# Seven block products in place of eight for the last matrix products, with the value products one step later and the loads of weights moved

## The reference

```
x  = attention(q, k, v)            # 8 heads of 64, a band of 96 keys and 8 global ones, bias by distance
x  = sum over 2 of 4 experts e:    # gate * softmax(causal, (x wq[e]) (x wk[e])') (x wv[e]) wo[e]
u  = x + (x' U V)'                 # rank 32, mixes the 768 tokens
out = u + relu(u w_ch1) w_ch2      # 512 -> 2048 -> 512
```

## Time and profile before

| | us |
|---|---|
| median of 3 runs (lowest, highest) | 459.03 (458.44, 459.3) |
| the profiled execution: its own time | 458.41 |
| its span, first to last instruction | 456.6 |
| PE busy, share of the span | 442.3 (97%) |
| DVE, ACT, POOL busy | 190.8, 167.1, 173.1 |

### The profile page before, as it was taken

How to read it: one execution, slowest core, us unless ns; L and a number is a source line. 1 busy time by engine, 2 the same in 40 slices (tenths; PEclk the granted TensorE clock), 3 DMA queues, 4 the chain that set the end, 5 groups by cost and what they waited for, 6 DMA issues and landing times.

```text
span 456.6 us, 8488 instructions
## 1 busy us (share of the span) xinstructions
PE 442.3 (97%) x3194; PEld 368.0 (81%) x3194; DVE 190.8 (42%) x616; ACT 167.1 (37%) x452; POOL 173.1 (38%) x243
## 2 busy tenths in 40 slices
PE   4999999999999999998999999999999999999996
PEld 3677777887787887767998888888888888888885
DVE  5799989455632733544352222212223122222112
ACT  4888788232553654656430111110112111111102
POOL 2667766924961365775212122222112111222210
PEclk9999999999999999999999999999999999999999
DMA  8899950110020011110102011111111032311003
GB/s 257 257 244 298 299 161 1 51 45 2 1 94 0 2 47 47 47 48 1 47 10 61 24 46 46 41 31 46 47 46 47 0 93 92 93 46 47 25 1 138
DMA packets 29949, 33.47 MB, mean 73 GB/s; under 512 B 9204, under 2 KB 19444, under 8 KB 29908
## 3 DMA queue, kind: packets, MB, share of 16 engines
q1 hardware_dynamic: 29474, 32.40, 24.0%
q10 hardware_dynamic: 434, 0.52, 0.3%
HBM read 29.77 MB, written 3.15 MB: 72 GB/s over the span
## 4 chain that ended last, share of the span: by engine, by line
PE 89%; DVE 4%; issue 3%; ACT 2%; DMA 1%; SPq 0%; POOL 0%; DVEq 0%; ACTq 0%
PE ps_s L1220 27%; PE ps_o L1220 25%; PE ps_t L1220 12%; PE ps_s L1451 5%; PE ps_o L1484 4%; PE ps_t L1467 4%; PE ps_o L1272 3%; PE ps_s L1239 3%; PE ps_t L1252 3%; DVE probT L865 1%; PE ps_o L1396 1%; ACT prob L604 1%; DMA kT<-in_k 1%; DVE prob L847 1%; DVE smin L847 0%
## 5 line engine op out<-in xcount | busy, mean ns | idle before, releaser
L492 POOL TENSOR_TENSOR fl<-fraw,fh 128x512 fp32r<-128x512 f32 x32 | 41.4, 1292 | 177.9 <-DVE fh L1162 177.9
L604 ACT ACTIVATE prob<-prob,smin 128x256 f32<-128x256 f32 (+3 forms) x144 | 77.7, 540 | 36.4 <-DVE smin L847 36.0
L796 ACT ACTIVATE hidh<-ps_o 128x768 fp32r<-128x768 f32 x32 | 26.0, 813 | 175.9 <-PE ps_o L1220 175.9
L1203 DVE SCALAR_TENSOR_TENSOR hidl<-ps_o,hidh 128x768 fp32r<-128x768 f32 x32 | 30.7, 958 | 92.6 <-ACT hidh L796 92.6
L541 POOL TENSOR_SCALAR prob<-prob,sinv,one 128x256 f32<-128x256 f32 (+1 forms) x96 | 50.6, 542 | 22.4 <-DVE sinv L878 22.4
L567 POOL TENSOR_SCALAR prob<-prob,sinv,gate 128x128 f32<-128x128 f32 (+5 forms) x48 | 34.0, 717 | 51.6 <-DVE sinv L898 51.5
L1220 PE MATMUL ps_s<-hidh,fl 128*128 128x512 f32 x128 | 50.4, 394 | 0.0
L1220 PE MATMUL ps_s<-hidl,fh 128*128 128x512 f32 x128 | 50.2, 392 | 0.0
L1220 PE MATMUL ps_s<-hidh,fh 128*128 128x512 f32 x128 | 49.7, 388 | 0.0
L1162 DVE CAST fh<-fraw 128x512 fp32r<-128x512 f32 x32 | 14.4, 450 | 66.8 <-PE ps_t L1220 66.8
L1220 PE MATMUL ps_o<-xh,w_late 128*128 128x512 f32 (+1 forms) x160 | 41.6, 334 | 0.0
(11 more groups left out here) (182 smaller groups left out, 978.3 us busy)
## 6 DMA issues: line engine op xcount, KB each, us to landing
fraw<-in_w SPq DMA_DIRECT2D x32, 256.0 KB, 2.7
wraw<-in_w SPq DMA_DIRECT2D x8, 512.0 KB, 3.4
kT<-in_k SPq DMA_DIRECT2D x16, 224.0 KB, 4.1
vN<-in_v SPq DMA_DIRECT2D x8, 384.0 KB, 4.9
out<-prob SPq DMA_DIRECT2D x12, 256.0 KB, 2.8
qT<-in_q SPq DMA_DIRECT2D x7, 384.0 KB, 3.8
vB<-in_v SPq DMA_DIRECT2D x8, 192.0 KB, 4.8
kT<-in_k SPq DMA_DIRECT2D x7, 128.0 KB, 3.9
```

The costliest lines, as they stand in the source:

```text
L492: return pool.tensor_tensor(lo, raw, hi.bitcast(F32), ALU.subtract)
L604: act.activation(prob_s, prob_s, ACT.Exp, bias=smin[:, col:col + 1], scale=-1.0, accum_out=ssum[:, col:col + 1]).then_inc(done, 1)
L796: act.activation(hidh[:, f % 2, :], ps_o[:, 0:S], ACT.Relu).then_inc(hidh_done, 1)
L1203: dve.scalar_tensor_tensor(hidl[:, f % 2, :], ps_o[:, 0:S], 0.0, hidh[:, f % 2, :].bitcast(F32), ALU.max, ALU.subtract).then_inc(hidl_done, 1)
```

## The change

**The block products.** The 512 x 128k by 128k x tokens product behind `second` and `whole` is cut in 2 x 2 blocks of weights (a11 to a22, 256 x 256 elements seen as 128 rows x 256) and of inputs (b11 to b22: 128 rows x 256 tokens), and done by Winograd's form of Strassen's scheme: 7 block products instead of 8, with 4 sums of weights (s1 to s4) and 4 sums of inputs (t1 to t4) made beforehand, and 7 sums of results behind. The 1536 tokens go through in three parts of 512 (the middle one spans the two batches). Each part has 9 "pairs" g: first wo with op, then 8 pairs of hidden blocks. Seven PSUM banks hold the seven products through a part; `ps_o[0:512]` is left for one hidden block.

For each pair and engine, in the order of its program:

- SP loads 512 KB of w2 (or wo) into `fraw` once the low parts of the pair two before are done.
- DVE: `weights_combined(g+2)`, four additions or subtractions 128 x 256 from `fraw` to `fraw`; `hidden_combined(g+1)`, four of 128 x 256 from `hraw` (or `o32`) to `t_raw`; `hidden_lo(g+1)`, 128 x 768; `combined_lo(g+1)`, 128 x 1024. In the last pair of a part it makes the six sums of 128 x 512 out of PSUM in place of `hidden_lo`.
- ACT: relu of two hidden blocks, 128 x 512 each, out of PSUM; `hidden_hi`, 128 x 768; `weights_hi(g+2)`, 128 x 1792; `combined_hi(g+1)`, 128 x 1024.
- POOL: the low parts of the seven weight blocks, one subtraction of 128 x 1792; and `sum_22`, one addition of 128 x 512 for a part.
- PE: hidden block (g+1, 0); two products; hidden block (g+1, 1); five products. A product is six matmuls of 256 columns. Products with a t block wait for `combined_lo`. In the first and the last pair of a part the order is END_ORDER.

**Attention.** `values` comes one step later (d-4), x with it, and the loop is one step longer. wk is loaded behind the third pair's keys and values, together with wq and wv; constants behind the fifth pair; wk, wq for the second heads and wo behind the last. POOL splits wk and wq between divisions (SPLIT_AT) and no longer before the first; ACT and DVE no longer split wq. POOL no longer splits wo, which now goes through the pairs.

```diff
+TOKENS, BLOCK = 512, 256
+PARTS = B * S // TOKENS
+PAIRS = FT // 2 + 1
+PRODUCTS = {1: ("a11", "b11"), 2: ("a12", "b21"), 3: ("s4", "b22"), 4: ("a22", "t4"), 5: ("s1", "t1"), 6: ("s2", "t2"),
+            7: ("s3", "t3")}
+ORDER, END_ORDER = (1, 2, 3, 5, 7, 6, 4), (1, 2, 6, 7, 5, 3, 4)
+SPLIT_AT = {13: 0, 16: 1, 19: 2, 22: 3}
...
 # SP
+                if g >= 2:
+                    sp.wait_ge(al_done, g - 1)
...
 # POOL
+                    if d in SPLIT_AT:
+                        split_weight(SPLIT_AT[d])
...
+            def sum_22(c):
+                pool.wait_ge(sum_step, SUMS * c + 3)
+                pool.wait_ge(copy_done, 2 * c + 2)
...
+                pool.tensor_tensor(y22, u3, c5, ALU.add).then_inc(y22_done, 1)
+            for g in range(N_PAIR):
+                pool.wait_ge(ah_done, g + 1)
+                lo_of(fraw[:, g % 2, 1:8, :], a_hi[g % 3], a_lo[g % 3]).then_inc(al_done, 1)
+                if g > PAIRS and g % PAIRS == 1:
+                    sum_22(g // PAIRS - 1)
+            sum_22(PARTS - 1)
 # ACT
+            for g in range(N_PAIR):
+                if last_of_part(g):
+                    copy_of(g // PAIRS, 1, c1)
+                    if g + 1 < N_PAIR:
+                        combined_hi(g + 1)
+                    copy_of(g // PAIRS, 5, c5)
+                    if g + 2 < N_PAIR:
+                        weights_hi(g + 2)
+                else:
+                    hidden_out(g + 1, 0)
+                    hidden_out(g + 1, 1)
+                    hidden_hi(g + 1)
+                    if g + 2 < N_PAIR:
+                        weights_hi(g + 2)
+                    combined_hi(g + 1)
 # DVE
+            def weights_combined(g):
+                a21, a11, a22, a12, s1, s2, s3, s4 = (fraw[:, g % 2, n, :] for n in range(8))
+                dve.wait_ge(f_in[g % 2], 16 * (g // 2 + 1))
+                dve.tensor_tensor(s1, a21, a22, ALU.add).then_inc(s_step, 1)
+                dve.tensor_tensor(s3, a11, a21, ALU.subtract).then_inc(s_step, 1)
+                dve.wait_ge(s_step, 4 * g + 1)
+                dve.tensor_tensor(s2, s1, a11, ALU.subtract).then_inc(s_step, 1)
+                dve.wait_ge(s_step, 4 * g + 3)
+                dve.tensor_tensor(s4, a12, s2, ALU.subtract).then_inc(s_step, 1)
...
+            def combined_lo(g):
+                dve.wait_ge(bth_done, g + 1)
+                dve.tensor_tensor(bt_lo[g % 2], t_raw, bt_hi[g % 2].bitcast(F32), ALU.subtract).then_inc(btl_done, 1)
...
+            for g in range(N_PAIR):
+                if g + 2 < N_PAIR:
+                    weights_combined(g + 2)
+                if g + 1 < N_PAIR:
+                    hidden_combined(g + 1)
+                if not last_of_part(g):
+                    hidden_lo(g + 1)
+                    combined_lo(g + 1)
+                else:
+                    sum_11(g // PAIRS)
+                    if g + 1 < N_PAIR:
+                        combined_lo(g + 1)
+                    other_sums(g // PAIRS)
 # PE
-                    if d >= 3:
-                        values(d - 3)
+                    if d >= 4:
+                        values(d - 4)
...
+            for g in range(N_PAIR):
+                order = END_ORDER if g % PAIRS in (0, PAIRS - 1) else ORDER
+                ahead = not last_of_part(g)
+                if ahead:
+                    hidden(g + 1, 0)
+                pe.wait_ge(al_done, g + 1)
...
+                for k, n in enumerate(order):
+                    if k == 2 and ahead:
+                        hidden(g + 1, 1)
+                    last = product(g, n)
```

More of the change, by code:

```diff
@@ L770, in _ @@
                 first_mixed_hi(n)
+            weights_hi(0)
             w01_hi(4)
@@ L773, in _ @@
             w01_hi(5)
+            combined_hi(0)
             mixed_hi(0)
@@ L776, in _ @@
             w01_hi(6)
+            weights_hi(1)
             w01_hi(7)
[L779 to L799, removed]
+            for g in range(N_PAIR):
[13 more added lines that the diff above has]
+                    combined_hi(g + 1)
         @block.vector
@@ L932, in _ @@
                 head_bias(0)
-                for d in range(N_DUO + 4):
+                for d in range(N_DUO + 5):
                     if 3 <= d < N_DUO + 3:
@@ L1176, in _ @@
             t3_lo(1)
+            hidden_combined(0)
             w01_lo(5)
@@ L1179, in _ @@
             mixed(1)
-            f_hi(0)
+            combined_lo(0)
+            weights_combined(1)
             w01_lo(6)
@@ L1606, in _ @@
-            hidden(0)
-            whole(0)
-            for f in range(B * FT):
-                if f + 1 < B * FT:
-                    hidden(f + 1)
-                second(f)
-                if f == FT - 1:
-                    whole(1)
+                w = slice(f * P, (f + 1) * P)
+                (b0, first), (b1, last) = tokens(c, 0), tokens(c, 1)
+                pieces = ([(b0, slice(first.start, last.stop), ps_o[:, 0:TOKENS])] if b0 == b1 else
+                          [(b0, first, ps_o[:, 0:BLOCK]), (b1, last, ps_o[:, BLOCK:TOKENS])])
@@ new lines, in product @@
+            def product(g, n):
+                c, j = divmod(g, PAIRS)
+                a, b = PRODUCTS[n]
+                if j == 0:
+                    empty(c, n)
+                if b[0] == "t":
+                    pe.wait_ge(btl_done, g + 1)
+                    x = B_SLOTS[b] - 3
+                    mh, ml = bt_hi[g % 2][:, x, :], bt_lo[g % 2][:, x, :]
+                elif j:
+                    pe.wait_ge(b1l_done, hidden_before(g) + 1)
+                    x = B_SLOTS[b]
+                    mh, ml = b1_hi[g % 2][:, x, :], b1_lo[g % 2][:, x, :]
+                else:
+                    mh, ml = (op_block(x, c, int(b[1]) - 1, 2 - int(b[2])) for x in (oph, opl))
+                for m in range(2):
+                    w = slice(m * P, (m + 1) * P)
+                    last = split_product(banks[n][:, m * BLOCK:(m + 1) * BLOCK],
+                                         [(a_hi[g % 3][:, A_SLOTS[a], w], a_lo[g % 3][:, A_SLOTS[a], w], mh, ml)],
+                                         start=j == 0 and m == 0, stop=last_of_part(g), skip_group_check=True)
+                return last
@@ new lines, in _ @@
+            for g in range(N_PAIR):
+                order = END_ORDER if g % PAIRS in (0, PAIRS - 1) else ORDER
[3 more added lines that the diff above has]
+                pe.wait_ge(al_done, g + 1)
+                if g % PAIRS == 0:
+                    pe.wait_ge(opl_done, OP_PIECES[1] if g else OP_PIECES[0])
+                for k, n in enumerate(order):
+                    if k == 2 and ahead:
+                        hidden(g + 1, 1)
+                    last = product(g, n)
+                    if not ahead:
+                        last.then_inc(acc_done, 1)
+                    elif n == order[-1]:
+                        last.then_inc(pair_done, 1)
```

378 lines of the change are left out of this document (212 added, 166 removed).

## The result

| | before | after |
|---|---|---|
| median (lowest, highest) | 458.77 (458.44, 459.3) | 482.68 (482.57, 483.52) |
| ratio, 95% interval | | 1.0536 (1.0515 to 1.0557) |
| span of the profiled execution | 456.6 | 480.9 |

Forecast was 487.4 us, in a range of 462 to 497.

What follows compares the result with a forecast made beforehand. PE bound the kernel before; exclusion between DVE and POOL would bind the changed last stage. 458.4 + 29.8 (last stage) + 0.6 (tail) - 2.0 (attention) = 486.8, or 487.4 us as median; range 462 to 497 for 8 in 10.

Steps and rivals of the forecast that it cites:

- Exclusion: Last stage: DVE operations with two SBUF operands and POOL's SBUF-reading subtraction wait for each other's whole length; chance 0.70.
- The period: Each pair of the last stage: DVE's 4.97 us plus POOL's 4.0 give 8.95 us, against PE's 7.5 us of work.
- The named sign: Last stage, what would show the forecast right: a pair period of 8.9 to 9.0 us.
- The stage's start: Last stage's opening: combined_lo(1), behind two of POOL's pieces, ends 15.7 us after the stage begins.
- Boundary: Between two parts of the last stage: the two pairs around it take 20.7 us, counted twice.
- End: Last stage's close, without POOL work: 7.5 us from combined_lo of the last but one pair.
- The tail: After the last product: DVE's last two sums end 1.25 us behind it, adding 0.6 us.
- Attention: Attention stage: values a step later and less wk loading at the start, less POOL's splits: -2.0 us (bounds -4 and +2).
- PE stays the bound: Rival, last stage: DVE's two SBUF operands don't meet POOL's subtraction; stage 199.8 us, time 443.6 us; chance 0.15.
- PE's saving: Last stage's block products: seven for eight cuts PE's 147.7 us to 129.3, 18.4 us fewer.
- Tightly packed: Rival, last stage: only the elements exclude, fixed parts and dependent waits overlap; period 7.9 us, time 461 us; chance 0.09.
- Extra order cost: Rival, last stage: POOL gets in before DVE's steps, or PE's clock falls at boundaries; period 9.5 and more, 498 to 505; chance 0.06.

Runs made afterwards that it cites:

- run 1: Changed kernel with POOL's subtraction for the low weights replaced by three zero fills of the same 1792 elements for each pair: 444.01 us.
- run 4: Changed kernel with the low weights shared, POOL subtracting four of the seven blocks (1024 elements) and DVE three (768): 461.8 us.
- run 8: Changed kernel with low weights on DVE, except those in a part's last pair, left on POOL beside DVE's PSUM sums; steps at parts' ends reordered: 445.48 us.
- run 5: Kernel before, last stage unchanged, with both attention edits: value products a step later, and loads and splits moved: 456.21 us, ratio 0.9928.
- run 7: Kernel before with only the attention loads moved and POOL splitting wk and wq between its divisions: 459.48 us, ratio 1.0015.
- run 6: Kernel before with only the value products, and x behind them, one step later: 456.98 us, ratio 0.9978.
- run 3: Changed kernel with all low weights on DVE, and combined_hi before weights_hi on ACT, combined_lo before the low weights on DVE: 455.75 us.

## Why the prediction was right

The mechanism and its place were right. The sizes were each a little off, and two of the larger errors, attention and tail, partly cancelled. Step by step:

- *Exclusion.* Shown by run 1 against the kernel after, and by run 4 in a middle dose. It had been worked out from rows in which the one or the other operation met a third. That DVE's sums out of PSUM are spared was assumed; run 8 shows it.
- *The period*, 8.95 predicted, 8.81 measured. Around the pair shown, the `combined_lo` before it ends at 260.35 (255.72 + 4.63 in the trace), `hidden_lo` 3.79 later (forecast 3.83), POOL 3.93 after that (4.0), and the next `combined_lo` 1.08 after that (1.14). Twenty periods took 176.1 us for 179.0: 2.9 of the 4.7 us by which the forecast was high. The named sign, 8.9 to 9.0, was missed by as little, and so was PE's 80 to 85% (206.33 of 240.10 is 86%).
- *The stage's start*, 15.7 against 251.53 - 235.94 = 15.6. *Boundary*, 20.7 against 333.27 - 313.15 = 20.1 and, at the second, 20.3: 1.0 us. *End*, 7.5 against 475.85 - 468.05 = 7.8. The stage is 239.9 for a forecast of 243.6.
- *The tail*, +0.6 predicted. After PE's end (475.85) 5.05 us follow, before 3.45: +1.6. This term was 1.0 short. The last sum ends 1.5 us behind the last product where I had 1.25, and from there 3.5 us pass where it was 2.8: SP issues the part's last three stores one behind another (1.44 us from 476.81, the last at 477.7, 0.3 behind the last sum), which I had left out.
- *Attention*, -2.0 predicted. The last stage begins at 235.94 in place of 239.38: -3.4. That is one execution. In the profiled executions of runs 1 to 5 and 8, which have the same attention code, the first matmul of that stage starts at 237.62, 236.16, 238.07, 236.09, 237.81 and 236.16; before it was at 239.22. Against that one trace of the kernel before the gain is 1.2 to 3.3 us (235.94 in the kernel after), 2.4 in the mean of the seven, and the forecast lies inside. The trace of the kernel after is at the far end of it. Run 5 shows that PE then stands for nothing from 20 to 94 us, where it stood for 2.2, and the rest of the 3.4 lies before and around that window. In the ratio of run 5, 0.9928, it is 3.3 us, by its medians 2.8. The 1.0 us that it put on POOL's splits between divisions shows in run 7 (stands of 3.0 for 2.2) and not in run 5 (0.0). The prediction had also credited nearly all of it to the value products alone, with the later loads at 0; in the trace of run 6 the keys' wait of 2.0 us shows that they need each other.
- *"The DMA doesn't bind"*, *"POOL's splits of wo cost nothing"*: no wait in the trace speaks against either.

Sum: -3.4 + 26.1 + 1.6 = +24.3, and the spans differ by 480.9 - 456.6 = 24.3. Of the 4.7 us between forecast and time, 3.7 are the stage and 1.4 attention, less 1.0 of the tail, and 0.6 had been added for the median, which the kernel after's profiled execution (482.70) did not lie below.

The rivals. *PE stays the bound* at 443.6: false as the change is made, but it is what the change gives once POOL's reads go (444.01 in run 1). Its last stage takes 199.8 us, from 237.62 to 437.41, as that rival's sum said. So the count of PE's saving was right too, and rival "the seven products themselves cost more" falls. *Tightly packed*, a period of 7.9: false, the fixed parts and the dependent sums do not overlap with POOL's time. *Extra order cost*: one half of it came about. PE stands for over 3 us at each boundary, and its clock falls behind that. The windows of the kernel after there (length, PE's busy time, the clock third from the end):

```profile
312.00:313.00 1.00, 0.00 (x0) 0.00 (x0) 1.00 (x1) 0.00 (x0) 0.07 (x1) 1.00 0.00 0
313.00:314.00 1.00, 0.79 (x3) 0.79 (x4) 1.00 (x4) 0.00 (x0) 0.00 (x0) 0.51 0.40 143
...
315.00:316.00 1.00, 1.00 (x7) 1.00 (x6) 0.97 (x3) 0.00 (x0) 0.00 (x0) 0.50 0.02 8
316.00:317.00 1.00, 1.00 (x9) 1.00 (x9) 0.69 (x2) 0.88 (x1) 0.00 (x0) 0.79 0.00 0
317.00:318.00 1.00, 1.00 (x11) 1.00 (x10) 0.79 (x1) 1.00 (x3) 0.00 (x0) 1.00 0.00 0
```

For some 3.2 us PE has half its clock, so it loses about 1.6 us of work. No cost of it shows: the chain from 313.15 to 333.27 has DVE's and ACT's pieces and none of PE, and the boundary came out shorter than forecast.

What stays open: why executions of the same attention code differ before 20 us. In the profiled execution of run 5 (456.97, the longest of its five) the first value products of the chain start at 20.11 us, in the kernel after at 17.88; the five executions of run 5 lie 1.8 us apart. Open too is what else, beside the longer round, makes up the 7.7 us of run 3.

## What to carry to other kernels

- Before work is shared out over DVE and POOL, count DVE's instructions with two SBUF operands and POOL's that read SBUF as one resource. DVE's cast, with one such operand, stood beside POOL's subtraction too. If the sum of both is above the bound engine's time, the faster engine should take the work, even though it is the busier one: 448 us for 483 here, by moving POOL's 4.0 us to 2.0 of DVE.
- What POOL keeps goes beside DVE's work out of PSUM, where run 8 had it at no cost to either.
- When two engines feed each other once in each round, the loop through both has a length of its own. Moving the thing that PE needs soonest to the front lengthened it from under 7.5 to 7.67 us, past PE's, and the run with that order was 7.7 us slower.
- A load that never made anyone wait may do so as soon as its consumer gets faster; price the two edits together.
- A term of 2 or 3 us can't be read from one execution of each kernel when executions of the same code lie 2 us apart.

## What the runs showed of the hardware

- A POOL memset of 128x1792 fp32 takes 1.60 us and does not hinder DVE's two-operand subtraction (1.23 us with POOL busy beside it); POOL's subtraction of that size takes 4.0 us and holds it until its end.
- DVE's sums of 128x512 with one operand in PSUM take 0.69 us beside POOL's subtraction, which takes 4.05 beside them: neither stands (run 8).
- A waiting instruction is shown as busy from its start, so the 26 `combined_lo` of the last stage's window show 110 us where 26 x 1.22 would be 32: some 78 of DVE's 226 us are stands in this line alone. The shortest time in the line's row (1.22 beside a median of 4.63) gives it away.
- PE's granted clock was 0.50 (1.2 GHz) for some 3.2 us behind a stand of 3.2 us, at both boundaries, and full (2.4 GHz) before and after it; the short stands of about 1 us in each pair left it at 1.00.
